# A convolution and two feed-forward layers on one core: the start is rearranged (two products on GpSimd, halves of the first weights, halo rows from two queues)

## The reference

```python
# _attn_ref: x [2, 4096, 192], weight_gen [2, 4096, 8 heads, 7 taps]
w = exp(weight_gen - max over taps);  w = w / (sum over taps + 1e-9)
out[b, s, head, :] = sum over k of w[b, s, head, k] * x_padded[b, s + k, head, :]   # 6 zero rows in front
# _moe_ref, then _moe2_ref, on [8192, 192]; w_in [192, 2048], w_out [2048, 192]
h = x @ w_in;  g = maximum(0.01 * h, h);  y = g @ w_out
h = y @ w_in2; r = maximum(h, 0);         out = (r * r) @ w_out2
```

## Time and profile before

| what | value |
|---|---|
| median of three runs | 1132.85 us |
| the profiled execution's own time | 1133.32 us |
| its span, first to last instruction | 1131.5 us |
| mean granted TensorE clock | 0.999 |
| PE busy | 1125.0 us, 99% |
| DVE busy | 868.8 us, 77% |
| ACT busy | 654.5 us, 58% |
| POOL busy | 3.8 us, 11 instructions |

### The profile page before, as it was taken

The page is one execution under the profiler, slowest core; times in us unless marked ns, Lnnn a source line. Parts: engine busy times, 40 slices in busy tenths (PEclk is TensorE's granted clock), DMA queues, the critical chain, the costliest instruction groups (busy, mean ns, idle before and its releaser), DMA issues.

```text
span 1131.5 us, 22864 instructions
## 1 busy us (share of the span) xinstructions
PE 1125.0 (99%) x10096; PEld 1103.0 (97%) x10096; DVE 868.8 (77%) x1066; ACT 654.5 (58%) x785; POOL 3.8 (0%) x11
## 2 busy tenths in 40 slices
PE   9999999999999999999999999999999999999998
PEld 7888999999999999999999999999999999999998
DVE  8888786877868787687877869778697786875575
ACT  5765646565564664655556465655656646566564
POOL 1000000000000000000000000000000000000000
PEclk9999999999999999999999999999999999999999
DMA  7311001010000101001010010100101001000001
GB/s 194 102 46 40 9 8 40 15 41 10 25 21 15 40 14 42 1 15 40 15 40 3 13 40 15 40 5 12 41 15 40 9 8 39 15 1 15 1 1 29
DMA packets 65058, 31.61 MB, mean 28 GB/s; under 512 B 53190, under 2 KB 62532, under 8 KB 64960
## 3 DMA queue, kind: packets, MB, share of 16 engines
q1 hardware_dynamic: 64960, 30.16, 10.2%
HBM read 23.84 MB, written 6.29 MB: 27 GB/s over the span
## 4 chain that ended last, share of the span: by engine, by line
PE 97%; DVE 1%; ACT 1%; SPq 0%; DMA 0%; issue 0%; DVEq 0%
PE h_pair L967 45%; PE y_main_psum L1012 30%; PE y_rest_psum L1016 20%; PE y_rest_psum L908 1%; PE h_pair L946 0%; PE h_pair L915 0%; DVE g_lo L753 0%; DMA raw_w_in<-in_moe_w_in_dram 0%; DVE tap_product L588 0%; SPq L290 0%; DVE u L625 0%; ACT g_hi L442 0%; ACT g L446 0%; PE y_main_psum L915 0%; ACT w_in_parts L377 0%
## 5 line engine op out<-in xcount | busy, mean ns | idle before, releaser
L967 PE MATMUL h_pair<-x_parts,w_in_parts 64*128 64x512 f32 x4590 | 568.1, 386 | 0.5 <-issue 0.5
L967 PEld LDWEIGHTS h_pair<-x_parts,w_in_parts 64*128 64x128 f32 x4590 | 515.2, 184 | 8.8 <-issue 0.9
L1012 PE MATMUL y_main_psum<-g_hi,w_out_parts 64*128 64x512 f32 x2040 | 448.6, 387 | 0.0
L753 DVE TENSOR_TENSOR g_lo<-g,g_hi 128x1024 fp32r<-128x1024 f32 x255 | 311.8, 1223 | 120.6 <-ACT g_hi L454 86.1
L1012 PEld LDWEIGHTS y_main_psum<-g_hi,w_out_parts 64*128 64x128 f32 x2040 | 241.2, 184 | 3.4 <-issue 0.3
L442 ACT ACTIVATE g_hi<-h_pair 128x1024 fp32r<-128x1024 f32 x128 | 131.7, 1029 | 190.7 <-PE h_pair L967 190.6
L454 ACT ACTIVATE g_hi<-g 128x1024 fp32r<-128x1024 f32 x127 | 134.8, 1061 | 170.6 <-DVE g L744 170.6
L1016 PE MATMUL y_rest_psum<-g_lo,w_out_parts 64*128 64x512 f32 x1020 | 223.7, 386 | 0.0
L1016 PE MATMUL y_rest_psum<-g_hi,w_out_parts 64*128 64x512 f32 x1020 | 223.6, 386 | 0.0
L1012 PE MATMUL y_main_psum<-g_lo,w_out_parts 64*128 64x512 f32 x1020 | 223.6, 386 | 0.0
L744 DVE SCALAR_TENSOR_TENSOR g<-h_pair,u 128x1024 f32<-128x1024 f32 x127 | 155.2, 1222 | 57.1 <-ACT u L448 56.6
(11 more groups left out here) (103 smaller groups left out, 448.2 us busy)
## 6 DMA issues: line engine op xcount, KB each, us to landing
x_window<-in_x_dram SPq DMA_DIRECT2D x14, 960.0 KB, 4.6
out_dram<-raw_w_in SPq DMA_DIRECT2D x360, 16.0 KB, 1.5
raw_w_out<-in_moe_w_out_dram SPq DMA_DIRECT2D x16, 192.0 KB, 3.2
tap_logits<-in_weight_gen_dram SPq DMA_DIRECT2D x16, 112.0 KB, 4.6
raw_w_in<-in_moe_w_in_dram SPq DMA_DIRECT2D x8, 192.0 KB, 4.3
raw_w_in<-in_moe_w_in_dram SPq DMA_DIRECT2D x24, 64.0 KB, 3.8
x_window<-in_x_dram SPq DMA_DIRECT2D x1, 768.0 KB
x_window<-in_x_dram SPq DMA_DIRECT2D x4, 141.8 KB
```

Source lines behind the costliest of these rows:

```text
L753: dve.tensor_tensor(GL[n % 4][:, :, :], gate[n % 2][:, :, :], GH[n % 4][:, :, :].bitcast(fp32), ALU.subtract).then_inc(glo_ready, 1)
L967: last = pe.matmul(h[:, i, :], w[r, slot, a, c], v[r, slot, b, :], start=first, stop=end)
L1012: return pe.matmul(ym[rows][:, :], w[r, c], g[r, i, :], start=start, stop=stop)
```

## The change

The diff does six things:

1. The products of taps 5 and 4 of chunk 0 move from DVE to GpSimd. DVE keeps five. PE takes the products in the order 6, 3, 5, 2, 1, 4, 0 (numbers are taps).
2. For chunk 0, DVE writes the tap weights twice: the two taps of GpSimd into SBUF, all seven into a free PSUM bank, from which its own products read them.
3. The addition of 1e-9 goes. `tap_exp` has an eighth column that holds 1e-9, and the sum runs over eight columns. Every chunk's softmax has five operations instead of six.
4. The halo rows are loaded in transfers of 48 and 15 rows instead of 63; the near half from SP, the far half from ACT, ahead of its first activation. SP waits for the far half before it issues the logits of chunk 1.
5. `w_in` piece 0 is split by tile: the first tile (128 columns) before `first_up`, the second after the spreads. `up` 1 now waits for the second.
6. The high rest of chunk 0's `x_parts` is copied by DVE instead of ACT; the spreads and low parts on DVE, and the products of `first_up`, are in another order. `softmax(1, 1)` (`tap_shifted` of chunk 1) moves behind the spreads.

```diff
+    POOL_TAPS = (5, 4)
+    TURN_ORDER = (0, 3, 1, 4, 5, 2, 6)
+    DVE_FIRST = [i for i in range(K) if FIRST_OPS[i][1] not in POOL_TAPS]
-        tap_exp = sb("tap_exp", [P, TH, K])
+        tap_exp = sb("tap_exp", [P, TH, K + 1])
+        first_tap_w = hb[1][:, 1, 0:TH * K].rearrange("p (a k) -> p a k", k=K)
+        HALO_ROWS = [(start + p, rows) for start in (0, BOOT) for p, rows in ((1, 48), (49, BOOT - 49))]
...
             load_first_taps(0)
             load_first()
             load_in_piece(0)
+            sync.wait_ge(far_loaded, NEAR_FAR)
             load_first_taps(1)
...
+            pool.wait_ge(pool_weights, 1)
+            pool.wait_ge(first_loaded[0], 16)
+            pool.wait_ge(near_loaded, NEAR_FAR)
+            for t in POOL_TAPS:
+                pool.tensor_tensor(FIRST[...], xwin[0][:, t * D:(t + TPC) * D]..., tap_w[:, :, t]..., ALU.mult).then_inc(pool_product, 1)
...
+            for p, rows in HALO_ROWS:
+                act.dma_start(xwin[0][p:p + rows, 0:HALF], ...).then_inc(far_loaded, 16)
             exp_of(0)
-            in_hi(0)
+            first_tiles_hi(0, 1)
             x_hi_main(0, PAIR[("first turn",)])
-            x_hi_rest(0, PAIR[("first turn",)])
             spread_hi_main(0)
             spread_hi_rest(0)
+            first_tiles_hi(1, JP)
             exp_of(1)
             in_hi(1)
...
-            first_products(range(K))
-            in_lo(0)
-            for i in range(2):
-                softmax(1, i).then_inc(conv_op, 1)
+            first_products()
+            softmax(1, 0).then_inc(conv_op, 1)
+            first_rest()
+            first_tiles_lo(0, 1)
             x_lo_main(0, PAIR[("first turn",)])
+            spread_lo_main(0)
             x_lo_rest(0, PAIR[("first turn",)])
-            spread_lo_main(0)
             spread_lo_rest(0, (turned_taken, 1))
+            softmax(1, 1).then_inc(conv_op, 1)
+            first_tiles_lo(1, JP)
...
+                if n == 1:
+                    pe.wait_ge(in_lo_done, 1)
```

More of the change, by code:

```diff
@@ L250, in load_first @@
                                bass.AP(x_flat.tensor, 0, [[TPP * D, P], [1, TPC * D]])).then_inc(first_loaded[0], 16)
[L251 to L259, removed]
+                for p, rows in HALO_ROWS:
+                    sync.dma_start(xwin[0][p:p + rows, HALF:2 * HALF],
+                                   bass.AP(x_flat.tensor, p * TPP * D - HALF, [[TPP * D, rows], [1, HALF]])
+                                   ).then_inc(near_loaded, 16)
             def load_second():
@@ L377, in in_hi, with first_tiles_hi @@
                 act.activation(WI[q // PIECES][:, :, 0, c:c + CP], raw_in[q % 2][:, :, :], ACT.Copy).then_inc(in_hi_done, 1)
+            def first_tiles_hi(a, b):
+                act.wait_ge(in_loaded[0], 64)
+                c = slice(a * P, b * P)
+                act.activation(WI[0][:, :, 0, c], raw_in[0][:, :, c], ACT.Copy).then_inc(in_hi_done if a else first_in_hi, 1)
             def out_hi(q):
@@ L386, in exp_of @@
                 act.wait_ge(conv_op, before(k) + EXP + 1)
-                act.activation(tap_exp[:, :, :], tap_shift[:, :, :], ACT.Exp).then_inc(exp_done, 1)
+                act.activation(tap_exp[:, :, 0:K], tap_shift[:, :, :], ACT.Exp).then_inc(exp_done, 1)
             def x_hi_main(s, pair):
@@ L395, in x_hi_rest @@
             def x_hi_rest(s, pair):
-                if s < 2:
+                if s == 1:
                     rest = X[s % 2][:, 1, 0, :].rearrange("p (a c) -> p a c", a=2)
-                    last = act.activation(rest, y_main_pair[:, :, 0:QC] if s == 0 else hb[pair][:, :, QC:2 * QC], ACT.Copy)
+                    last = act.activation(rest, hb[pair][:, :, QC:2 * QC], ACT.Copy)
                 else:
@@ L925, in turn_first @@
                 rest = [ym[i][:, 0:QC] for i in range(2)]
[L926 to L927 removed]
+                for i in TURN_ORDER:
+                    if i in DVE_FIRST:
+                        pe.wait_ge(conv_op, SOFT + DVE_FIRST.index(i) + 1)
+                    else:
+                        pe.wait_ge(pool_product, POOL_TAPS.index(FIRST_OPS[i][1]) + 1)
                     done = turn_product(FIRST[FIRST_OPS[i][2]], main, rest, True, i == 0, i == K - 1)
@@ L992, in first_up @@
                 product(2, 1, 0)
+                pe.wait_ge(turned_taken, 1)
+                product(1, 0, 1)
                 pe.wait_ge(x_lo_spread, 2)
```

104 lines of the change are left out of this document (71 added, 33 removed).

## The result

The changed kernel took 1134.74 us (median of 20 runs, 1134.35 to 1137.01), the kernel before 1133.16 in the same comparison (20 runs, 1132.35 to 1134.61): ratio 1.0016, interval 1.0010 to 1.0023. That is +1.6 us, which the forecast called "the same" and put at +0.9. The profiled execution's span grew from 1131.5 to 1133.2 us, +1.7, at a granted clock of 1.0; it accounts for the difference. Sixteen of the 20 runs lie between 1134.35 and 1134.95; the other four took 1135.91 to 1137.01 at a mean granted clock of 0.998, and none of these was profiled.

What follows compares the result with a forecast made beforehand. PE was 99% busy, so only its waits counted, set by when ACT reaches `exp` of chunk 1 and `g_hi`. 0.88 + 0.1 (logits) - 0.05 (softmax) = +0.9 us, 1133.8; range 1131.9 to 1135.6, forecast's own 1133.1 to 1134.9.

Steps and rivals of the forecast that it cites:

- Softmax: Chunk 0's softmax on DVE: dropped addition, wider sum and extra small `tap_weights` together make it 0.05 us earlier.
- Far halo: ACT's four early issues: halo packets delay the logits 0.1 us (0 to 0.4); the table load stays covered by 0.3.
- Products: Chunk 0's products: DVE's five end near 10.1 instead of 11.83; GpSimd's two take 2.0 us each, costing nothing up to 2.4.
- PE's pace: PE's transposes of chunk 0's products: 0.785 us per product and zero pair, so the transposed chunk is only 0.29 earlier.
- DVE's queue to `exp`: DVE's work after the transposed chunk: `tap_shifted` ends at 15.92, so `exp` of chunk 1 and `g_hi` start 0.88 us later.
- The way to 40.83: From `g_hi` through `w_out` piece 0, SP and `w_in` piece 3 to chunk 1's transposes: everything follows by 0.88 us.
- Piece 2: `w_in` piece 2 leaves SP only after the second tile's split: 0 to 0.6 us on ACT, taken as none.
- the blocking one: Rival at the start: GpSimd and DVE products block each other, total +3.4 us, 1136.2; chance 0.12, shared with slower GpSimd.
- the faster one: Rival at PE's transposes of chunk 0: PE keeps DVE's pace, chunk another 1.2 us earlier, 1131.4 to 1132.5; chance 0.15.
- the absorbed one: Rival at PE's wait at 40.83: piece 3's slow issue runs undisturbed, the wait goes, total -0.15 us, 1132.7; chance 0.2.
- A falling clock: Rival at the start: PE's clock falls in its gaps between 12.6 and 16.5 us; chance 0.03.
- The change doesn't do what it says: Rival at the start: logits or `exp` late by up to 1.1 us, first products no sooner, total +2.0, 1134.9; no separate chance.

Runs made afterwards that it cites:

- both edits: The changed kernel with the far halo rows issued by SP and `tap_shifted` of chunk 1 directly behind its `tap_max`: 1133.08 us against 1133.07 for the kernel before.
- the first of the last three versions: Both edits, `w_in` piece 0 split whole before the transposed chunk, far half from ACT behind its table load in 63-row transfers: 1135.35 us against 1133.04 for the kernel before.

## Why the prediction was right, and what it mis-sized

The forecast mechanism is the one that happened: the products stop being the limit, PE paces the start, `exp` of chunk 1 sits behind `tap_shifted`, and the delay runs through `g_hi`, `w_out`, SP and piece 3 to the transposes. In numbers, step by step:

- Softmax, -0.05: shown as about nothing. From `tap_max` to the first product 2.78 us with both edits, against 2.79 before. In the changed kernel it took 2.87, 0.08 of it in a `tap_shifted` of 0.47; with the same transfers beside it that instruction took 0.41 and 0.39 in two other versions, so why stays open.
- Far halo, +0.1 for the logits, with 0.4 as the upper end: wrong in size, by 0.9 of the sum. It was +0.99. This is the step that failed. No row had such packets beside the logits, and I sized them by the length of one issue, which says nothing about the time of its packets. The other half of that step, the table load in time for `exp`, held by luck: each issue cost 0.50 instead of 0.36, over the 0.42 from which I had put the cover at an end. The table was in at 4.03, 0.3 after the 3.71 at which `exp` had started before; only because the logits were later still did it hold nothing. SP's new wait for the far half, put at nothing, was 0.47 us (6.20 to 6.67), and nothing on the chain waited for it.
- Products: GpSimd 1.54 us each, inside 0.7 to 3.0, and free of cost as forecast. The Trainium skill's figure (GPSIMD Engine Reference, "Elementwise — side-by-side cycle accounting"), which gave an estimate of 1.7, is nearer than my 2.0. GpSimd's products did not start with the small weights (done at 6.39) but at 7.29. GpSimd's row above names what they waited for, the near half of the halo: its last transfer, issued at 3.04, landed 4.1 us later, and 3.0 later with the far half on SP, where GpSimd started at 6.2. The forecast left this landing out; it cost nothing.
- PE's pace, six steps of 0.785: 4.73 us between first and last pair against 4.71 forecast; the gain over before 0.27 against 0.29. Undoing GpSimd's part alone cost 0.21.
- DVE's queue to `exp`: 3.86 us from the ready chunk instead of 3.61. Each of the two spreads held the next instruction off for 0.45 where I had 0.34 (0.42 less the overlap of 0.08): behind a spread there is no overlap, and the next starts 0.03 later instead. The trace of the kernel before has it already, beside the row of 15.11 in the earlier trace rows:

```profile
14.66 0.42 DVE L686 CAST x_parts<-x_parts 64x512 fp32r<-64x512 f32 x1
...
15.56 0.39 DVE L578 TENSOR_REDUCE tap_sum<-tap_exp 128x32 f32<-128x224 f32 x1
```

- The way to 40.83, taken as rigid: it gave back 0.42. The slow issue took 1.62 us instead of 1.89 (-0.27), the transfer 2.75 instead of 2.83, and 0.07 went between `g_hi` and the split. Piece 2 held nothing, as taken.

The measured sum: +0.92 at the first pair, -0.27 for the pace, +1.44 in DVE's queue (forecast 1.17), -0.42 on the way, +1.7. The forecast's error of 0.8 is the logits' 0.9 and the queue's 0.27, less 0.42. That the last helped is luck: nothing in the forecast asked for it. Of the marks set beforehand, the spacing of the pairs, `exp` directly behind `tap_shifted` and PE's wait before the transposes (0.7) held; the four times came 0.8 to 1.3 late (13.30, 17.16, 18.29 and 42.51 against 12.35, 15.9, 17.1 and 41.7). Of the rivals, the blocking one did not occur, since the weights lie in PSUM; the pairs were no closer than 0.78, so the faster one fell; the slow issue moved along (1.62 us in the changed kernel, 1.71 with both edits), so the absorbed one had its 0.3 of it and not the whole. A falling clock, put at 0.03, can't be dismissed: four of the changed kernel's 20 runs had 0.998, against two of the 104 runs of the kernel before that stand in the experiments' comparisons. They left the median alone, and where the clock fell in them is not known; in the profiled execution PE stood 0.9 us ahead of the first transposed product, at 7.83, without losing it. "The change doesn't do what it says" was half right: logits were late by 1.0, the first product came at 6.73 instead of 5.66, and the measured +1.6 lies between the forecast's +0.9 and its +2.0, somewhat nearer to it. It had stood as the upper end of the forecast, with no chance of its own.

## What to carry over

A second queue for a load saved the issuer's time, not the transfers': SP reached its first weights at 3.50 instead of 5.29, and the logits came 1.0 late. Before moving one, list what is in flight then and what waits for it first, and price it by the length of those packets. Here four small early transfers from another engine cost a microsecond at the one load on which the kernel starts. And an engine relieved of work gives back only as much as the next one's pace allows, here 0.2 us of 1.7. Once PE is the pace, a start that leaves it idle may lose its clock as well, as three executions here did: read the granted clock of the stretch before blaming the engine that was late. Last, the order of what is queued behind the handover decided more than the relief.

## What was not expected of the hardware

- The 128x224 logits land 2.1 us after their issue when SP alone issues, 3.0 to 3.3 us with four small transfers issued by ACT from 0.74 on.
- A halo issue on SP costs 0.45 in the split of 48 and 15 rows and 0.36 with 63 rows, whether ACT issues too (1.79 for four) or not (1.79 and 1.74). On ACT it is 0.50.
- Two SBUF inputs on DVE beside a GpSimd product: 2.26 us instead of 0.9 for one DVE product of 128x768, 2.08 instead of 1.54 for GpSimd's.
- PE's granted clock fell to 0.5, its lower level, for 3.4 to 6.8 us in three profiled executions, after PE had stood 2.0 to 2.2 us waiting for products (0.9 in the changed kernel and 1.2 in the first of the last three versions, where it did not fall). A transposed product with its zero pair then took 1.4 us instead of 0.79.
- One issue of a weight piece takes 1.2 to 1.9 us where its fellows take 0.6, in most of the chains above but not at the same issue. In each of these traces the queue list shows an instruction fetch of 16 KB over the slow issue: in the kernel before one from 21.6 for the issue at 21.90, in the changed kernel one from 24.8 for that at 24.58. That the fetch is the cause is not shown.
